# Third batch chosen one slot sooner, pair 1 read without the table, weight pieces 2 and 3 loaded later

## What is computed

```python
# 1: B, H, S, D = 4, 8, 768, 48
for t in range(S):
    cur = np.einsum('bhd,bhe->bhde', u[None] * kt, vt)
    y[:, :, t] = np.einsum('bhd,bhde->bhe', rt, state + cur)
    state = wt[:, :, :, None] * state + np.einsum('bhd,bhe->bhde', kt, vt)
# 2: 3072 tokens of 384, 8 experts of 384x1024 and 1024x384
expert_idx = np.argmax(logits, axis=1)          # one expert for each token
h = np.maximum(x[mask] @ w1[e], 0.0)
out[mask] = gate_w[mask, None] * (h @ w2[e])
# 3: d_ff = 2048
h = x @ w_in
g = h * np.tanh(sp)                             # sp = softplus(h)
return g @ w_out
```

## Time and profile before

| | us |
|---|---|
| median of 3 runs (938.64 to 941.72) | 941.7 |
| profiled execution | 938.3 |
| its span | 936.1 |
| TensorE busy | 879.5 (94%) |
| VectorE, ScalarE, GpSimd busy | 553.8, 540.5, 475.2 |

### The profile page before, as it was taken

One profiled execution on the slowest core, in us unless ns is written; L12 is line 12 of the kernel. 1 busy time (PEld: TensorE's weight loads), 2 busy tenths in 40 slices (PEclk: granted clock), 3 DMA queues, 4 the chain that ended last, 5 costly groups with the idle time before them and its releaser, 6 DMA issues. The chain is left out here.

```text
span 936.1 us, 17518 instructions
## 1 busy us (share of the span) xinstructions
PE 879.5 (94%) x5639; PEld 780.5 (83%) x5639; DVE 553.8 (59%) x1075; ACT 540.5 (58%) x1090; POOL 475.2 (51%) x273
## 2 busy tenths in 40 slices
PE   2899999769999999999999899999999999999994
PEld 2688887648999989898998699899898899898893
DVE  5799998463343433334345766665766666666653
ACT  2355554224444443444447887777887887877881
POOL 3576787458763826876200434533533633633643
PEclk9999999779999999999999999999999999999998
DMA  9579772555444435544312000200200101000000
GB/s 223 144 219 272 197 208 85 174 180 158 141 138 134 145 112 178 168 146 142 118 37 90 36 1 1 68 0 0 68 0 11 57 0 34 34 0 1 35 1 34
DMA packets 31283, 88.66 MB, mean 95 GB/s; under 512 B 3856, under 2 KB 16112, under 8 KB 31216
## 3 DMA queue, kind: packets, MB, share of 16 engines
q1 hardware_dynamic: 18832, 65.17, 23.7%
q10 hardware_dynamic: 9312, 13.04, 4.2%
q0 software_dynamic: 3072, 9.59, 2.7%
HBM read 70.42 MB, written 17.36 MB: 94 GB/s over the span
## 5 line engine op out<-in xcount | busy, mean ns | idle before, releaser
L470 POOL TENSOR_TENSOR gl<-gg,gh 128x512 fp32r<-128x512 f32 x96 | 154.3, 1607 | 287.5 <-DVE gh L1068 287.5
L1058 DVE SCALAR_TENSOR_TENSOR am<-am,yz 128x512 f32<-128x512 f32 x96 | 70.7, 736 | 123.2 <-ACT am L647 123.2
L1344 PE MATMUL ps<-whi,gh 128*128 128x384 f32 x384 | 130.8, 341 | 3.2 <-POOL gl L470 3.2
L1346 PE MATMUL ps<-whi,gl 128*128 128x384 f32 x384 | 129.4, 337 | 0.0
L1345 PE MATMUL ps<-wlo,gh 128*128 128x384 f32 x384 | 129.4, 337 | 0.0
L1264 PE MATMUL ps<-xh,whi 128*128 (+1 forms) x288 | 116.5, 405 | 3.1 <-DVE gg L1064 3.1
L1265 PE MATMUL ps<-xl,whi 128*128 (+1 forms) x288 | 113.9, 395 | 0.0
L1266 PE MATMUL ps<-xh,wlo 128*128 (+1 forms) x288 | 113.9, 395 | 0.0
L424 POOL TENSOR_TENSOR wlo<-raw,whi 128x1536 fp32r<-128x1536 f32 x32 | 112.1, 3503 | 2.7
L656 ACT ACTIVATE tn<-ps 128x512 f32<-128x512 f32 x96 | 57.3, 596 | 57.6 <-PE ps L1266 55.0
L431 POOL TENSOR_SCALAR whi<-raw 128x1536 fp32r<-128x1536 f32 x32 | 47.5, 1485 | 84.1 <-PE ps L1266 79.1
(11 more groups left out here) (156 smaller groups left out, 1948.8 us busy)
## 6 DMA issues: line engine op xcount, KB each, us to landing
raw<-in_wall SPq DMA_DIRECT2D x40, 768.0 KB, 4.6
rkb<-in_rk SPq DMA_DIRECT2D x16, 672.0 KB, 6.6
expert_out<-yo ACTq DMA_DIRECT2D x31, 194.0 KB, 3.6
xg<-expert_rows ACTq DMA_DIRECT2D x30, 198.0 KB, 3.0
decay<-in_wdec SPq DMA_DIRECT2D x16, 338.6 KB, 3.9
vt_in<-in_vt SPq DMA_DIRECT2D x16, 336.0 KB, 7.0
vb<-in_vv SPq DMA_DIRECT2D x16, 288.0 KB
xin<-expert_out SPq DMA_DIRECT2D x5, 776.0 KB, 4.4
```

What stands on the lines that cost most here:

```text
L470: nc.gpsimd.tensor_tensor(gl[:, f % 4], gg[:, :], gh[:, f % 4].bitcast(F32), ALU.subtract).then_inc(s_gl, 1)
L1058: nc.vector.scalar_tensor_tensor(out=am[:, par], in0=am[:, par], scalar=0.75, in1=yz[:, par], op0=ALU.add, op1=ALU.mult).then_inc(s_rr, 1)
L1344: pe.matmul(o, high, hi, start=(f == 0), stop=False)
L1346: last = pe.matmul(o, low, hi, start=False, stop=(f == FT2 - 1))
```

## The change

- `CHOOSE_AT` is (9, 12) instead of (9, 13). VectorE chooses batch 3 at slot 12, ahead of product(15), TensorE counts in slot 13, and `ranks_out(1)`, `positions(1)` and `hold(1)` run in slot 14 around the masks of slot 15.
- `hold(1)` writes a second flag: whether the first expert has at least 256 rows in the first three batches. It also fills a second set of columns of `tab` with constants. If the flag is set, pair 1 reads these; if not, it waits for the table as before (`s_tab`).
- The rows of pair 1 are fetched by SyncE instead of ScalarE, behind the scatters of two groups.
- On SyncE the fetch for pair 0 now stands ahead of pieces 2 and 3 and waits for a product of slot 14; the fetch for pair 1 stands behind them.
- ScalarE's first_high(2) and first_high(3) and VectorE's first_low(2) and first_low(3) move into the first two pairs. VectorE's order becomes: x_low(0), table, x_low(1), first_low(2), h_low(0), first_low(3), wait for all scatters, gate of pair 0.
- TensorE's order becomes: turn x(0), hidden(0), turn h(0), turn x(1), hidden(1), project(0), turn x(2), turn h(1), wait for the table, hidden(2).
- GpSimd waits for the clearing, the positions and the rows once for a group and no longer before each scatter.

```diff
-CHOOSE_AT = (9, 13)
+CHOOSE_AT = (9, 12)
...
-        for j in range(2, PIECES):
-            sp.wait_ge(s_lo, j + 1)
-            piece(j, j % 2)
         sp.wait_ge(s_held, 1)
         rest = sp.value_load(held[0:1, 0:1], min_val=1, max_val=2)
         sp.wait_ge(s_scat[0], 16 * tiles_of(0)[1])
         sp.wait_ge(s_all, rest)
+        sp.wait_ge(s_bon, 2 * (SLOTS - 1))
         sp.dma_start(xg[:, 0], xs[0:P, :]).then_inc(s_xg[0], 16)
+        for j in range(2, PIECES):
+            sp.wait_ge(s_lo, j + 1)
+            piece(j, j % 2)
+        sp.wait_ge(s_held, HELD)
+        rest = sp.value_load(held[0:1, 1:2], min_val=1, max_val=2)
+        off = sp.value_load(held[0:1, 2:3], min_val=0, max_val=T_EARLY)
+        for g in range(2):
+            sp.wait_ge(s_scat[g], 16 * tiles_of(g)[1])
+        sp.wait_ge(s_all, rest)
+        sp.wait_ge(s_tab, rest)
+        sp.wait_ge(s_bon, 2 * SLOTS)
+        t = sp.value_load(tab[1:2, bass.ds(off + T_ROW, 1)], min_val=0, max_val=E * N - P)
+        sp.dma_start(xg[:, 1], xs[bass.ds(t, P), :]).then_inc(s_xg[1], 16)
...
         def scatter(t):
-            pool.wait_ge(s_clear, 16 * E)
-            pool.wait_ge(s_rt, RT_ALL * (group_of(t) + 1))
-            pool.wait_ge(s_rows, 2 * PAIRS * (t // CH + 1) - 1 + t % CH // HALF)
+            if t == tiles_of(group_of(t))[0]:
+                group_ready(group_of(t))
...
-        act.wait_ge(s_held, 2)
-        rest = act.value_load(held[0:1, 1:2], min_val=1, max_val=2)
         x_high(0, 0)
         length(0, 0)
+        first_high(2)
         relu(0)
-        act.wait_ge(s_r, R_TAB)
-        for g in range(2):
-            act.wait_ge(s_scat[g], 16 * tiles_of(g)[1])
-        act.wait_ge(s_all, rest)
-        rows_in(1, 1)
         h_high(0)
         x_high(1, 1)
+        first_high(3)
         length_root(0, 0)
+        act.wait_ge(s_r, R_TAB)
         all_landed(act)
         rows_in(2, 0)
...
+            if g == 1:
+                nc.vector.tensor_scalar(held[0:1, 2:3], placed, float(2 * P), float(T_EARLY), ALU.is_ge, ALU.mult).then_inc(s_held, 1)
+                for k, v in ((T_ROW, P), (T_WAIT, PIECES // 2 + 2), (T_SLOT, SLOT[0])):
+                    nc.vector.memset(tab[:, T_EARLY + k:T_EARLY + k + 1], v).then_inc(s_held, 1)
...
+            if it == CHOOSE_AT[1] + 2:
+                ranks_out(1)
             if 0 <= it + 1 < SLOTS:
                 masks(it + 1)
-            if it - 2 in CHOOSE_AT and it == SLOTS - 1:
-                ranks_out(1)
+            if it == CHOOSE_AT[1] + 2:
                 positions(1)
                 hold(1)
...
+            if it == CHOOSE_AT[1]:
+                choose(1)
             if it + 3 < SLOTS:
                 product(it + 3)
-            if it == CHOOSE_AT[1]:
-                choose(1)
...
-        first_low(2)
         choose(len(GROUPS) - 1)
...
+        x_low(1, 1)
+        first_low(2)
         h_low(0)
-        x_low(1, 1)
+        first_low(3)
         all_landed(dve)
...
         turn_h(0)
+        pe.wait_ge(s_held, HELD)
+        rest = pe.value_load(held[0:1, 1:2], min_val=1, max_val=2)
+        off = pe.value_load(held[0:1, 2:3], min_val=0, max_val=T_EARLY)
+        pe.wait_ge(s_tab, rest)
+        turn_x(1, 1, 16)
+        hidden(1, 1, place_of(1, off), off)
+        project(0, SLOT[0])
+        turn_x(2, 0, 32)
+        turn_h(1)
         pe.wait_ge(s_r, R_TAB)
-        turn_x(1, 1, 16)
-        for p in range(1, NPAIR):
+        for p in range(2, NPAIR):
```

More of the change, by code:

```diff
@@ L74 @@
 T_ROW, T_WAIT, T_SLOT, T_OUT, T_ALL = range(5)
+T_EARLY = 5
+HELD = 6
 X_START, X_CAP, X_FIRST, X_SLOT = range(4)
@@ L107, in routed_kernel @@
     raw = at("raw", [P, 2, PCOLS])
-    tab = at("tab", [P, 5], I32)
+    tab = at("tab", [P, 2 * T_EARLY], I32)
     waits = at("waits", [P, E], I32)
-    held = at("held", [P, 2], I32)
+    held = at("held", [P, 3], I32)
     tok_i = at("tok_i", [P, BT], I32)
@@ L218, in routed_kernel @@
     s_all = sem("s_all")
+    s_tab = sem("s_tab")
     s_raw = [sem("s_raw0"), sem("s_raw1")]
@@ L246, in routed_kernel @@
     GA, GB = 3, 4
-    HIGH_AT = (SLOTS - 6, SLOTS - 5, SLOTS - 1, SLOTS)
+    HIGH_AT = (SLOTS - 6, SLOTS - 5)
     def chunks(ap):
@@ L411, in product_rk, with group_ready @@
             nc.gpsimd.tensor_tensor(kr[0:ROWS, par], rkb[0:ROWS, m % 3, 0], rkb[0:ROWS, m % 3, 1], ALU.mult).then_inc(s_kr, 1)
+        def group_ready(g):
+            if g == 0:
+                pool.wait_ge(s_clear, 16 * E)
+            pool.wait_ge(s_rt, RT_ALL * (g + 1))
+            pool.wait_ge(s_rows, 2 * PAIRS * GROUPS[g][1])
         def scatter(t):
-            pool.wait_ge(s_clear, 16 * E)
-            pool.wait_ge(s_rt, RT_ALL * (group_of(t) + 1))
-            pool.wait_ge(s_rows, 2 * PAIRS * (t // CH + 1) - 1 + t % CH // HALF)
+            if t == tiles_of(group_of(t))[0]:
+                group_ready(group_of(t))
             nc.gpsimd.indirect_dma_start(
@@ L587, in _ @@
                 states(it + 1)
-            for k in [k for k in range(PIECES) if HIGH_AT[k] == it]:
+            for k in [k for k in range(PIECES // 2) if HIGH_AT[k] == it]:
                 first_high(k)
@@ L738, in _ @@
         dve.sem_inc(s_mask, 3)
+        dve.sem_inc(s_tab, 1)
         dve.sem_inc(s_a, 2)
@@ L996, in _ @@
         assert step_of[0] + 1 == R_TAB
-        first_low(3)
+        dve.wait_ge(s_r, R_TAB)
+        dve.sem_inc(s_tab, 1)
         def gate_first(p, par):
@@ L1222, in _ @@
             if it == SLOTS - 2:
-                counts(CHOOSE_AT.index(it - 1))
                 updates(it + 1)
@@ L1267, in product, with place_of, hidden @@
             return last
-        def place_of(p):
-            return pe.value_load(tab[p:p + 1, T_SLOT:T_SLOT + 1], min_val=0, max_val=WCOLS) if p else SLOT[0]
-        def hidden(p, par, at_):
-            pieces = pe.value_load(tab[p:p + 1, T_WAIT:T_WAIT + 1], min_val=0, max_val=PIECES * E) if p else PIECES // 2 + 2
+        def place_of(p, off=0):
+            return pe.value_load(tab[p:p + 1, bass.ds(off + T_SLOT, 1)], min_val=0, max_val=WCOLS) if p else SLOT[0]
+        def hidden(p, par, at_, off=0):
+            pieces = pe.value_load(tab[p:p + 1, bass.ds(off + T_WAIT, 1)], min_val=0, max_val=PIECES * E) if p else PIECES // 2 + 2
             pe.wait_ge(s_xtl, p + 1)
```

## The result

| | before | after |
|---|---|---|
| median of 5 runs each, side by side, us | 941.7 (937.96 to 944.03) | 946.78 (946.26 to 948.26) |
| ratio | | 1.0057 [1.003, 1.0083] |
| profiled execution | 938.3 | 946.26 |
| its span | 936.1 | 944.1 |

The change makes the kernel slower by 0.3 to 0.8%; between the medians lie 5.1 us. The forecast was 935.0 with a range to 941, so the prediction was wrong in size and sign; the rival that came true in kind is (c), given at 943.8 with a chance of 0.14.

The account below looks back on a forecast made before the run. Only the passage from recurrence to pair loop (168 to 220.75 us) could give time, TensorE being busy elsewhere. Hole 3 3.25, choice 0.1, masks -0.1 gave 3.3 us: 938.3 to 935.0, range 924 to 941.

Parts of the forecast that it names:

- (c): Rival, slower: sixteen scatters in a row hold TensorE's signals, slot 15's states at 186.4 instead of 177.6; 943.8 us, chance 0.14.
- hole 1: TensorE idle 4.88 us from 173.1, waiting for ScalarE's first state of slot 15; forecast to stay unchanged.
- Rival (a): Hole 1 closes too, as piece 2 and pair 1's fetch move; up to 10.2 us more, 925.0 us, chance 0.30.
- The remark on the transfers: From 169 to 172 scatters stood still behind piece 2 on the transfer queues; added nothing to the sum.
- Hole 3: TensorE's wait from pair 0's hidden turning (203.74) to pair 1's hidden product (209.17); 3.25 us to be gained.
- hole 2: The choice of the last batch between slot 15 and pair 0; shortened by almost nothing, 0.1 us in the sum.
- My choice of full clock: TensorE in the first pairs: a hidden product takes 4.3 us at full clock, leaving 3.25 us of gain.
- The case of the low clock for all of pair 1's product: Half clock makes that product 8.6 us, pair 2 starts at 220.0; gain only 0.7 us.
- Choice one slot sooner: VectorE's choice of batch 3, 2.0 us, moves into a wait of 1.92; at most 0.1 us shows.
- Waits once for a group: GpSimd's scatter step of 1.28 may shorten to no less than 0.97; 0 to 0.3 a scatter, nothing taken.
- Later pieces: Weight pieces leave later, GpSimd's splits from 212, 5 us spare; cost nothing, without that cover 1 to 2 us.
- Fetch for pair 1: SyncE fetches pair 1's rows near 188, once batches 1 to 3 have landed, without the table.

Follow-up runs that it names:

- f2: The version after with `tab` 8 columns wide instead of 10, so 32 bytes as before: 943.71 us, ratio 1.0033 to before.
- e6: The version after, unedited, run again on chip 1: 946.71 us, ratio 1.0062 to before.
- g2: The version after with `tab` 8 columns wide and at most four scatters in flight: 944.03 us, ratio 1.0035 to before.
- g4: The version before with at most three scatters in flight: 936.52 us, ratio 0.995 to before.
- g3: The version after with `tab` 8 columns wide, at most two scatters in flight, the last group without limit: 935.07 us, ratio 0.9936 to before.
- e4: The version after with pieces 2 and 3 again loaded ahead of the fetch for pair 0, chip 5: 930.75 us, ratio 1.0001 to before.
- e1: The version after with batch 3's scatters held back until slot 15's chunk products, chip 5: 929.47 us, ratio 0.9981 to before.
- h2: The version after with `tab` 8 columns wide and seven short pauses of GpSimd fills between scatters: 932.1 us, ratio 0.9903 to before.
- h3: The version before with one long pause of eight GpSimd fills ahead of scatter 6: 935.68 us, ratio 0.9941 to before.
- e2: The version before with at most two scatters in flight, chip 5: 943.23 us, ratio 1.0139 to before.
- e3: The version after with at most two scatters in flight, chip 5: 938.66 us, ratio 1.0083 to before.
- g1: The version after with `tab` 8 columns wide and at most three scatters in flight: 943.8 us, ratio 1.0029 to before.
- h1: The version after with `tab` 8 columns wide and one long pause of eight GpSimd fills ahead of scatter 8: 939.83 us, ratio 0.9985 to before.

## Why the prediction was wrong, step by step

**The step that failed** is "I forecast 935.0, with hole 1 unchanged". It took the lateness at slot 14 as a fixed property of that place. It comes with GpSimd's run of scatters, which the change lengthens from ten to sixteen; the text of (c) had the mechanism in the main, its place and its price. (c) put the state at 186.4, 8.8 later, less 3.3: +5.5. Measured were the end of the run at 184.98, the second state at 185.29, and +6.9 to the last logits less 1.3: +5.6. That the sums agree is luck, as both terms of (c) were some 2 us too large. Nor is a spell as long as its run: the first state came sooner than before, at 176.10 instead of 177.62, and the longer run added a second hold behind it. Other profiles of the unbroken sixteen have the second state at 182.40 (f2, 4.0 ahead of the end of the run), 184.55 (e6, 0.3 ahead) and 186.25 (g2, 0.4 ahead). Against (c) I had set that the second spell of before began 15 us after its run. That fact holds, but it was an argument on when a spell begins, not on when it ends, and both spells of before ended just behind a run. What picks the moments at which a spell begins and ends is still open.

**Not in the sum at all:** the placement of tiles, 2.4 to 2.5 us of stage 3. The diff had it in plain sight, `tab` growing from 20 to 40 bytes, and I counted only instructions and waits. (c)'s 943.8 and this term give 946.3; the profiled execution took 946.26, which is in part the same luck.

**Rival (a)** was wrong. It had the pile behind piece 2 as the cause; piece 2 left at 179.44, after the first state, and the spell was there without it. The remark on the transfers stands as an observation of those 3 us, but it is no rule (in g4 from 171.6 to 172.6 scatters moved 0.27 MB and the piece 0.10), and it has no part in the spells.

**Hole 3** was right in kind and mis-sized: 0.6 us instead of 3.25 in the pair of profiles. The other 0.75 of the 1.3 lies in hole 2, between the last logits and pair 0's product, for which the sum had 0.1. Three things took the rest of hole 3. The wait before pair 1's product closed by 2.7 instead of 3.7, as TensorE stood 0.96 and 1.25 us around the turning. Pair 0's product and its turning took 0.66 longer. From pair 1's product to pair 2's it took 13.03 instead of the forecast 12.05. My choice of full clock failed: the granted clock fell at 214.3 and came back at 217.8, so the product took 219.12 - 213.27 = 5.85 instead of 4.3. And turn_x(2) waited 0.36 us for its rows, which were asked for at 219.54 and not "as before": 9.0 us behind the turning of pair 0's hidden rows, where the forecast had 8.4. Other pairs of kernels give the change without the spell at slot 15 1.5 us (g3 and g4), 2.0 and 3.3 (e4 and e1), 3.6 (h2 and h3), 7.0 (e2 and e3). The sum lies within these, but no two of them differ by the change alone. The case of the low clock for all of pair 1's product, for which I had a gain of only 0.7 and which I set aside, is the nearest to the 0.6 measured.

**Choice one slot sooner:** free, as forecast; the scatters started at 163.03, where 164.6 was forecast, the positions were there at 169.65 and not 172.3, and slot 14's masks were not late. **Waits once for a group:** the step stayed 1.28 us with its gap of 0.30, the lower bound of the forecast. **Later pieces:** cost nothing, with less spare: splits from 219.3 instead of 212, for the last pieces left at 214.8 instead of 207 and 210; TensorE waited for no weights. **Fetch for pair 1:** 193.7 instead of 188, and still in time. In all, the loss was decided by a coupling between two engines that share no wait, and by an address; and the gain that was to pay for the change, 3.3 us, was 1.3 in this pair of profiles.

## What to carry to other kernels

When signals of one engine come late with no releaser in the trace, look at what another engine issues in that stretch and ask where each spell ends; a change that lengthens that run can lengthen the spell or add one. Try to break up long runs of indirect scatters on GpSimd with other work of its own, and test it on more than one chip: the pauses were tried on one only, and on chip 5 a limit in flight cost 8 us or more. When a diff changes the size of a tile, the addresses of all tiles behind it change too: compare the length of a stage that the change doesn't touch, and keep the old padding.

## What the runs showed of the hardware

- On three chips of four that were told apart (0, 1 and 7), and on the one first profiled or another like it, finished work of TensorE reaches ScalarE and VectorE up to 12.7 us late (g1) during an unbroken run of indirect scatters (one each 1.28 us). Some signals come through within the run (176.10 and 182.51 in after, 184.88 in h3), the others by 2.5 us behind its end, and 0.9 and 1.1 us into a pause (g4, h1); a wait of 1.25 us in g1 let none through. On the fourth (chip 5) a run of 22 held nothing, and before took 930.4 there instead of 939.6 to 942. What is held, and what differs between the chips, is not known.
- Number and traffic of the transfers don't decide it: signals were late with the DMA engines at 0.43 (after, 170 to 175) and came through at 0.91 with three scatters in flight (g4, 171.6 to 172.5).
- Behind a spell TensorE's own work is slow as well: after idle stretches of 5.07 and 7.13 us its granted clock was 0.50 from 185 to 190 in after.
- 32 bytes of shift in the tiles make the six blocks of stage 3 2.0 to 2.5 us longer out of 412, on the three chips on which both widths were profiled (1, 5 and 7). The cause is open.
- GpSimd's eight fills of 440 elements, each waiting for the one before it, took 4.14 us, 0.52 each; two took 1.00.
